# The first expert's weights: halves behind four tiles in place of whole units behind two

## The chip, the cores and the metric

The kernel runs on one core of a Trainium2 chip. The metric is the device time of one execution in microseconds (us), the median of several executions. TensorE (PE) multiplies matrices, VectorE (DVE) and ScalarE (ACT) work on elements, GpSimd (POOL) gathers rows, and SyncE (SP) issues nearly all DMAs. An engine runs its own instructions in the order in which they are written, and engines wait for each other and for DMAs on semaphores.

## The reference

Three blocks, one after the other; only the first and the beginning of the second bear on this change.

```python
    batch, n_heads, seq, head_dim = (4, 8, 576, 64)
    ...
    N, D, E, F = (2304, 512, 8, 1024)
    ...
    n_tokens, d_model, d_ff = (2304, 512, 1536)
    ...
    scores = scale * np.matmul(q, k.transpose(0, 1, 3, 2))
    gamma = 1.0 - 2.0 ** (-5.0 - np.arange(H, dtype=np.float32))
    ...
    Dmat = np.where(rel >= 0, gamma[:, None, None] ** rel[None, :, :], 0.0)
    ret = scores * Dmat[None, :, :, :]
    return np.matmul(ret, v).astype(np.float32)
...
    logits = x @ w_gate
    e_idx = np.argmax(logits, axis=1)
    ...
    for e in range(E):
        ...
        h = np.maximum(x[mask] @ w1[e], 0.0)
        ye = h @ w2[e]
        out[mask] = gate_w[mask, None] * eom[mask, e, None] * ye
...
    a = x @ w_a
    b = x @ w_b
    return (a * b @ w_out).astype(np.float32)
```

All data are float32. `w1` of one expert is 512 x 1024 (2 MB), `w2` of one expert 1024 x 512 (2 MB).

## The kernel before

**Stage 1 (about 0 to 112 us): decay attention and routing.** The 576 positions of each of the B = 4 batches are cut into C = 5 tiles: four of 128 rows and a last one of 64. Tile c of batch b is written (b, c) here. For each tile, SP loads q, k and v (pieces of 256 bytes, two DMAs each for q and k and one for v), DVE scales q and k by powers of the decay (`scale_qk`), PE turns them (`turn_qk`), multiplies them (`score`), DVE masks (`probs`), PE multiplies by v (`mix`) and carries a state to the next tile. The result x of the tile is turned back by `turn_x` together with the gate logits (`keep_logits` on DVE), copied to `x_tok` by ACT (`keep_x`) and stored to `x_tokens` in HBM by SP (`store_tile`). Batch 0 is written out; SP runs the loads of batches 1 to 3 in a loop over b = 0, 1, 2 which in each turn, for each c, stores (b, c), waits until `mix` of (b, c) is done (the buffers of tile c come free then), and loads (b + 1, c). The last batch's stores stand behind the loop. At tile (b, c), DVE scales (b, c + 2) and PE turns (b, c + 1), so the loads of a tile have some three tiles of time from their release to their use.

**The first expert's weights.** The expert that runs first is always expert 0, so that its 4 MB can be loaded during stage 1 into `land[0]`: 8 units of 512 KB, of which units 0 to 3 (kind 0) are w1 and units 4 to 7 (kind 1) are w2. `load_first(kind, i)` (called from line 616 on, the DMA is put down to line 598) waits until the load before it of the same kind has landed, by the semaphores `first_in`, and issues unit i of that kind. In turn b, a unit of w1 goes behind the loads of tile (b + 1, 3) and one of w2 behind those of (b + 1, 4); the last unit of each kind goes behind the loop and ahead of the last batch's stores. ACT rounds each unit to `w_hi` and DVE subtracts it to `w_lo` (`first_low`). The table `first_units` says where: ACT copies unit 0 in (1, 1), unit 4 in (1, 3), 1 and 5 in batch 2, and in the last batch unit 2 in (3, 1), 3 in (3, 2), 6 in (3, 3) and 7 at the very end of the stage. In a tile, this copy is ACT's last work, and the next instruction behind it is the copy of the next tile's turned q (`qT`, line 912), for which PE waits in `turn_x`.

**Stage 2 (121 to 347 us)** runs windows of tokens through the experts, with the next expert's weights loaded meanwhile; **stage 3 (to the end)** is the two-factor block with seven products for eight. Neither is touched. PE is busy in both almost all the time.

Of the kernel before, what the change touches and what calls it, by code (L numbers as in the profile page):

```python
# [35 lines left out]
def retention_moe_bilinear(nc, q, k, v, w_gate, w_output_gate, w1, w2, w_a, w_b, w_out, out):  # L36
# [11 lines left out]
    P = 128  # L48
    B, H, S, DH = q.shape
    D = H * DH  # L50
    N = B * S
    E, _, F = w1.shape
    F2 = w_a.shape[1]
    DC = D // P
# [4 lines left out]
    C = -(-S // P)  # L59
# [48 lines left out]
    UNIT = 1024  # L108
# [17 lines left out]
    with ctx:  # L126
# [6 lines left out]
        def sem(name):  # L133
            return ctx.enter_context(nc.semaphore(name))
# [38 lines left out]
        land = []  # L173
# [239 lines left out]
        first_in = [sem("first_up_in"), sem("first_down_in")]  # L413
# [69 lines left out]
        def after(b, c, n):  # L483

            return b + (c + n) // C, (c + n) % C

        def first_units(b, c, first, last):


            if first:  # L490
                return None
            if last:
                return {1: (2, 4), 2: (3, 5), 3: (6, 6)}.get(c)
            return {1: (b - 1, b * 2 - 2), 3: (b + (DC - 1), b * 2 - 1)}.get(c)
# [71 lines left out]
        def _(sp):  # L566
            from_q_k_v = ((q, q_in, q_in_done), (k, k_in, k_in_done), (v, v_in, v_in_done))

            def load_tile(b, c, which=from_q_k_v):
                r = ROWS[c]  # L570
                for src, dst, done in which:
                    rows = src.rearrange("b h s d -> s b h d")[c * P:c * P + r, bass.ds(b, 1)]
                    to = dst[0:r, c, :].rearrange("s (b h d) -> s b h d", b=1, h=H)
                    if src is v:
                        sp.dma_start(to, rows).then_inc(done[c], 16)  # L575
                    else:

                        for half in range(2):
                            sp.dma_start(to[:, :, half:H:2, :], rows[:, :, half * HP:half * HP + HP, :]).then_inc(done[c], 16)  # L579

            def store_tile(b, c):
                r = ROWS[c]
                sp.wait_ge(x_ready, b * C + (c + 1))
                sp.dma_start(x_dram[bass.ds(b * S + c * P, r), :], x_tok[0:r, c, :]).then_inc(x_stored[c], 16)

            def load_first(kind, i):

                sp.wait_ge(first_in[kind], i * 16 + 16)  # L590
                sp.sem_inc(alone_sp, 1)
                if kind == 0:
                    src = w1.rearrange("e (d p) f -> p (e d) f", p=P)[:, bass.ds(i, 1), :]
                    dst = land[0][:, bass.ds(i, 1), :]
                else:
                    src = w2.rearrange("e (g two p) n -> p (e g) two n", p=P, two=2)[:, bass.ds(i, 1), :, :]
                    dst = land[0][:, bass.ds(i + DC, 1), :].rearrange("p u (g n) -> p u g n", g=2)
                sp.dma_start(dst, src).then_inc(first_in[kind], 16)


# [8 lines left out]
            with sp.Fori(0, B - 1) as b:  # L609
                for c in range(C):  # L610

                    store_tile(b, c)
                    sp.wait_ge(mixed, b * C + (c + 1))
                    load_tile(b + 1, c)
                    if c >= C - 2:
                        load_first(c - (C - 2), b)
            for kind in range(2):
                load_first(kind, B - 1)
            for c in range(C):
                store_tile(B - 1, c)  # L620

# [286 lines left out]
        def _(act):  # L908
            def turn_qk(b, c):
                r = ROWS[c]  # L910
                act.wait_ge(q_turned, b * C + (c + 1))
                nc.scalar.copy(qT[:, c, :, 0:r], pq[:, :, 0:r]).then_inc(qT_ready, 1)
                act.wait_ge(k_turned, b * C + (c + 1))
                nc.scalar.copy(kT[:, c, :, 0:r], pk[:, :, 0:r]).then_inc(kT_ready, 1)

            def keep_state(b, c):
                act.wait_ge(state_done, b * (C - 1) + (c + 1))
                nc.scalar.copy(state[:], pstate[:]).then_inc(state_kept, 1)

            def keep_xT(b, c):  # L920
                r = ROWS[c]
                act.wait_ge(mixed, b * C + (c + 1))
                nc.scalar.copy(xT[:, :, 0:r].rearrange("p (h n) t -> p h n t", h=2), pout[:, :, 0:2, 0:r]).then_inc(xT_ready, 1)


            def keep_x(b, c):
                r = ROWS[c]
                act.wait_ge(logits_kept, b * C + (c + 1))
                act.wait_ge(x_stored[c], b * 16 + 16)
                for h, bank in enumerate(x_banks(b, c)):  # L930
                    ins = nc.scalar.copy(x_tok[0:r, c, 2 * h * P:2 * (h + 1) * P].rearrange("p (i n) -> p i n", i=2),
                                         bank[0:r, 0:2 * TURNED].rearrange("p (i n) -> p i n", i=2)[:, :, 0:P])
                ins.then_inc(x_ready, 1)
# [12 lines left out]
            def batch(b, first, last):  # L946
                for c in range(C):
                    if not (last and c == C - 1):
                        turn_qk(*after(b, c, 1))
                    if not (first and c == 0) and not (last and c == C - 1):  # L950
                        keep_x(*after(b, c, -1))
                    if c < C - 1:
                        keep_state(b, c)
                    keep_xT(b, c)
                    if last and c == C - 1:
                        keep_x(b, c - 1)
                    unit = first_units(b, c, first, last)
                    if unit:
                        u = unit[0]
                        if last:  # L960
                            act.wait_ge(first_in[u // DC], 16 * (u % DC) + 32)
                        else:
                            act.wait_ge(first_in[c // 3], b * 16 + 16)
                        act.sem_inc(alone_act, 1)
                        nc.scalar.copy(w_hi[0][:, bass.ds(u, 1), :], land[0][:, bass.ds(u, 1), :]).then_inc(hi_done, 1)

            batches(act, batch)
            keep_x(B - 1, C - 1)
            act.wait_ge(first_in[1], 16 * DC + 16)
            nc.scalar.copy(w_hi[0][:, UE - 1, :], land[0][:, UE - 1, :]).then_inc(hi_done, 1)  # L970


# [1177 lines left out]
```

## Time and profile before

| | |
|---|---|
| median of 3 runs | 775.74 us (773.78 to 776.17) |
| profiled execution | 770.1 us |
| its span, first to last instruction | 768.1 us |
| mean granted clock of TensorE | 0.995 of full speed |
| busy share of the span: PE, DVE, ACT, POOL | 98%, 63%, 36%, 10% |
| DMA, mean over the span | 220 GB/s, 168.81 MB |
| DMA, 0 to 160 us | 35.97 MB in 68445 packets, 59284 of them under 512 bytes |

The profile is one execution; its own time of 770.1 us is the span and 2.0 us around it. A row of the timeline below gives start, duration, engine, line, operation and tiles, the count of merged instructions, and in brackets how long the engine stood idle before it and whom the profile puts that down to. An instruction of SP that issues a DMA is shown with the time that the issue takes, not the transfer.

### The profile page before, as it was taken

How to read it: one execution, taken by the hardware profiler on the slowest of the kernel's cores; microseconds unless marked ns; L12 is line 12 of the kernel's file. 1: busy time of each engine (PE TensorE's matmuls, PEld its weight loads, DVE VectorE, ACT ScalarE, POOL GpSimd, SP SyncE). 2: the span in 40 equal slices, each digit the busy share in tenths (PEclk: the TensorE clock that was granted, in tenths of full speed). 3: DMA queues.
4: the chain of work that ended last, by engine and by line, in shares of the span. 5: the costliest groups of instructions: out<-in, count | busy, mean ns of one | idle time of the engine just before them, and what ended most of it. 6: DMA issues, size and time to landing. Idle time of an engine off the chain costs nothing.

```text
span 768.1 us, 14705 instructions
## 1 busy us (share of the span) xinstructions
PE 754.7 (98%) x5370; PEld 702.2 (91%) x5370; DVE 481.0 (63%) x925; ACT 275.8 (36%) x500; POOL 78.7 (10%) x108
## 2 busy tenths in 40 slices
PE   9999999999999999999999999999999999999996
PEld 6888868999999999999899999999999999999994
DVE  5678886577576676666567787547654555544371
ACT  4454543465464554533132343211321221221021
POOL 2000032101101110100011100301110030111003
PEclk9999999999999999999999999999999999999998
DMA  9989927397788789587732767875444476444402
GB/s 172 229 231 247 240 98 226 124 357 261 258 321 297 237 296 337 189 327 278 307 128 80 261 257 292 300 285 204 158 189 153 190 260 233 168 175 173 170 1 82
DMA packets 116630, 168.81 MB, mean 220 GB/s; under 512 B 63981, under 2 KB 83472, under 8 KB 116560
## 3 DMA queue, kind: packets, MB, share of 16 engines
q1 hardware_dynamic: 111149, 156.90, 60.4%
q0 software_dynamic: 4176, 10.92, 4.5%
q8 instruction: 41, 0.67, 0.4%
q10 hardware_dynamic: 1234, 0.07, 0.1%
q14 instruction: 30, 0.24, 0.1%
HBM read 131.34 MB, written 36.54 MB: 219 GB/s over the span
## 4 chain that ended last, share of the span: by engine, by line
PE 88%; SPq 5%; issue 2%; DVE 2%; DMA 1%; ACT 1%; POOL 0%; POOLq 0%; DVEq 0%; ACTq 0%
PE pz L2079 34%; PE po L2104 19%; PE py L2024 14%; PE pu L2013 9%; SPq L579 4%; PE pu L1995 4%; PE pu L2003 2%; PE px L1966 1%; PE pscore L1780 1%; PE pout L1850 1%; SPq L575 1%; PE pq L1803 1%; PE pk L1803 1%; PE pstate_bank L1836 1%; DMA x_blk<-x_tokens,slots 1%
## 5 line engine op out<-in xcount | busy, mean ns | idle before, releaser
L2079 PE MATMUL pz<-x_hi,w_hi 128*128 128x384 f32 x504 | 170.4, 338 | 0.3 <-DVE u L1639 0.3
L2079 PE MATMUL pz<-x_hi,w_lo 128*128 128x384 f32 x504 | 170.0, 337 | 0.0
L2079 PE MATMUL pz<-x_lo,w_hi 128*128 128x384 f32 x504 | 169.7, 337 | 0.0
L1639 DVE TENSOR_TENSOR u<-pz,p 128x384 f32<-128x384 f32 x72 | 40.1, 558 | 115.4 <-PE pz L2079 115.4
L2079 PEld LDWEIGHTS pz<-x_hi,w_hi 128*128 128x128 f32 x504 | 94.6, 188 | 3.3 <-DVE u L1639 0.6
L2079 PEld LDWEIGHTS pz<-x_lo,w_hi 128*128 128x128 f32 x504 | 94.8, 188 | 0.7
L2079 PEld LDWEIGHTS pz<-x_hi,w_lo 128*128 128x128 f32 x504 | 94.8, 188 | 0.0
L1080 ACT COPY p<-pz 128x384 f32<-128x384 f32 x36 | 17.3, 480 | 212.7 <-PE pz L2079 212.7
L2104 PE MATMUL po<-wo_hi,g_hi 128*128 128x512 f32 x216 | 84.3, 390 | 0.0
L2104 PE MATMUL po<-wo_hi,g_lo 128*128 128x512 f32 x216 | 84.3, 390 | 0.0
L2104 PE MATMUL po<-wo_lo,g_hi 128*128 128x512 f32 x216 | 84.2, 390 | 0.0
L2024 PE MATMUL py<-h_hi,w_hi 128*128 128x320 f32 (+6 forms) x256 | 80.2, 313 | 0.0
L2024 PE MATMUL py<-h_hi,w_lo 128*128 128x320 f32 (+6 forms) x256 | 77.5, 303 | 0.0
L2024 PE MATMUL py<-h_lo,w_hi 128*128 128x320 f32 (+6 forms) x256 | 77.4, 303 | 0.0
L1539 DVE TENSOR_TENSOR w_lo<-land,w_hi 128x1024 fp32r<-128x1024 f32 x56 | 68.5, 1223 | 10.7 <-ACT w_hi L1005 10.3
L1005 ACT CAST w_hi<-land 128x1024 fp32r<-128x1024 f32 x56 | 58.7, 1048 | 0.2 <-DMA land<-in_moe_w_dram 0.2
L2013 PE MATMUL pu<-x_hi,w_hi 128*128 128x320 f32 (+6 forms) x160 | 49.3, 308 | 0.0
L1095 ACT CAST g_hi<-g 128x384 fp32r<-128x384 f32 x72 | 33.6, 514 | 43.2 <-DVE g L1662 39.9
L2013 PE MATMUL pu<-x_lo,w_hi 128*128 128x320 f32 (+6 forms) x160 | 48.5, 303 | 0.0
L2024 PEld LDWEIGHTS py<-h_lo,w_hi 128*128 128x128 f32 x256 | 48.4, 189 | 0.0
L2013 PE MATMUL pu<-x_hi,w_lo 128*128 128x320 f32 (+6 forms) x160 | 48.4, 302 | 0.0
L2104 PEld LDWEIGHTS po<-wo_hi,g_lo 128*128 128x128 f32 x216 | 40.6, 188 | 8.5
(261 smaller groups left out, 1318.8 us busy)
## 6 DMA issues: line engine op xcount, KB each, us to landing
land<-in_moe_w_dram SPq DMA_DIRECT2D x64, 512.0 KB, 7.6
w_hi<-bilinear_weights SPq DMA_DIRECT2D x31, 896.0 KB, 4.6
w_lo<-bilinear_weights SPq DMA_DIRECT2D x31, 896.0 KB, 7.0
bilinear_weights<-w_hi SPq DMA_DIRECT2D x12, 896.0 KB, 10.1
bilinear_weights<-w_lo SPq DMA_DIRECT2D x12, 896.0 KB, 11.4
wo_land<-in_moe_w_out_dram SPq DMA_DIRECT2D x18, 512.0 KB, 3.9
q_in<-in_q_dram SPq DMA_DIRECT2D x32, 128.0 KB, 3.2
k_in<-in_k_dram SPq DMA_DIRECT2D x32, 128.0 KB, 3.3
```

What stands on the lines that cost most here:

```text
L579: sp.dma_start(to[:, :, half:H:2, :], rows[:, :, half * HP:half * HP + HP, :]).then_inc(done[c], 16)
L1005: nc.scalar.copy(w_hi[1 - s][:, u, :], land[1 - s][:, u, :]).then_inc(hi_done, 1)
L1080: nc.scalar.copy(p1[:], pz[n % 2][:, 0:T]).then_inc(z_kept_act, 1)
L1095: nc.scalar.copy(hi[:, MADE[i], :], g[:, MADE[i], :]).then_inc(g_hi_ready, 1)
L1539: nc.vector.tensor_tensor(w_lo[1 - s][:, u, :], land[1 - s][:, u, :], w_hi[1 - s][:, u, :], ALU.subtract).then_inc(lo_done, 1)
L1639: nc.vector.tensor_tensor(dst, pz[n % 2][:, 0:T], more, ALU.add).then_inc(z_kept_dve, 1)
L1803: last = nc.tensor.matmul(banks[h][0:r, second * P:second * P + TURNED], xT[:, d, 0:r], turn_w[:, h, (1 - second) * LG:(1 - second) * LG + ...
L1995: last = nc.tensor.matmul(pu[f][:, cols_of], w[s][:, d, at(f)], x_hi[:, d, cols_of], start=(d == 0 and w is w_hi), stop=False)
L2013: last = nc.tensor.matmul(pu[f % NPU][:, cols_of], w, m[:, d, cols_of], start=(d == 0 and n == 0), stop=(d == DC - 1 and n == 2))
L2024: last = nc.tensor.matmul(py[d][:, cols_of], w, m[:, f, cols_of], start=(f == 0 and n == 0), stop=(f == FF - 1 and n == 2))
L2079: ins = nc.tensor.matmul(pz[n % 2][:, 0:T], w, m, start=(k in FRESH and j == 0 and i == 0), stop=(j == DH2 - 1 and i == 2), skip_group_che ...
L2104: ins = nc.tensor.matmul(po[i][:], m[:, c, rows], w_, start=(q == 0 and f == 0 and n == 0), stop=(q == NQ - 1 and f == 1 and n == 2))
```

## The change

`load_first` gets a third argument and fetches half a unit: of a w1 unit the left or right 512 of its 1024 columns (so 2 KB a row in place of 4 KB), of a w2 unit one of its two groups of 128 rows (2 KB a row, as before). The halves of the two kinds of turn b go behind the loads of the tiles (b + 1, 1), (b + 1, 2), (b + 1, 3) and (b + 1, 4), and the last units follow behind the loop as four halves. Each half still waits for the one before it of its kind, so the second half of a unit now waits for the first half to land. The counts for which ACT waits are adapted; when and in which order ACT and DVE work on the units stays the same.

```diff
--- before.py
+++ after.py
@@ -585,16 +585,17 @@
 
 
 
-            def load_first(kind, i):
-
-                sp.wait_ge(first_in[kind], i * 16 + 16)
+            def load_first(kind, i, half):
+
+                sp.wait_ge(first_in[kind], i * 32 + (16 * half + 16))
                 sp.sem_inc(alone_sp, 1)
                 if kind == 0:
-                    src = w1.rearrange("e (d p) f -> p (e d) f", p=P)[:, bass.ds(i, 1), :]
-                    dst = land[0][:, bass.ds(i, 1), :]
+                    cols = slice(half * (UNIT // 2), (half + 1) * (UNIT // 2))
+                    src = w1.rearrange("e (d p) f -> p (e d) f", p=P)[:, bass.ds(i, 1), cols]
+                    dst = land[0][:, bass.ds(i, 1), cols]
                 else:
-                    src = w2.rearrange("e (g two p) n -> p (e g) two n", p=P, two=2)[:, bass.ds(i, 1), :, :]
-                    dst = land[0][:, bass.ds(i + DC, 1), :].rearrange("p u (g n) -> p u g n", g=2)
+                    src = w2.rearrange("e (g two p) n -> p (e g) two n", p=P, two=2)[:, bass.ds(i, 1), half, :]
+                    dst = land[0][:, bass.ds(i + DC, 1), :].rearrange("p u (g n) -> p u g n", g=2)[:, :, half, :]
                 sp.dma_start(dst, src).then_inc(first_in[kind], 16)
 
 
@@ -612,10 +613,11 @@
                     store_tile(b, c)
                     sp.wait_ge(mixed, b * C + (c + 1))
                     load_tile(b + 1, c)
-                    if c >= C - 2:
-                        load_first(c - (C - 2), b)
+                    if c >= 1:
+                        load_first((c - 1) // 2, b, (c - 1) % 2)
             for kind in range(2):
-                load_first(kind, B - 1)
+                for half in range(2):
+                    load_first(kind, B - 1, half)
             for c in range(C):
                 store_tile(B - 1, c)
 
@@ -958,15 +960,15 @@
                     if unit:
                         u = unit[0]
                         if last:
-                            act.wait_ge(first_in[u // DC], 16 * (u % DC) + 32)
+                            act.wait_ge(first_in[u // DC], 32 * (u % DC) + 48)
                         else:
-                            act.wait_ge(first_in[c // 3], b * 16 + 16)
+                            act.wait_ge(first_in[c // 3], b * 32 + 16)
                         act.sem_inc(alone_act, 1)
                         nc.scalar.copy(w_hi[0][:, bass.ds(u, 1), :], land[0][:, bass.ds(u, 1), :]).then_inc(hi_done, 1)
 
             batches(act, batch)
             keep_x(B - 1, C - 1)
-            act.wait_ge(first_in[1], 16 * DC + 16)
+            act.wait_ge(first_in[1], 32 * DC + 16)
             nc.scalar.copy(w_hi[0][:, UE - 1, :], land[0][:, UE - 1, :]).then_inc(hi_done, 1)
 
 
```

On SP, at the loads of tile (b + 1, 2) in the loop, the order before is this: line 575 is the v load that ends a tile (here of tile 1), line 584 the store of the next tile's x, and lines 579 and 575 its loads.

```order
L575 DMA v_in<-in_v_dram 128x8x64
L583 REGISTER_ALU
L584 ISA [waits x_ready]
L584 DMA x_tokens<-x_tok 128x512
L579 ISA [waits mixed]
L579 DMA q_in<-in_q_dram 128x4x64
L579 ISA
L579 DMA q_in<-in_q_dram 128x4x64
```

The order after, at the same place:

```order
L575 DMA v_in<-in_v_dram 128x8x64
L590 ISA
L599 ISA [waits first_up_in]
L599 DMA land<-in_moe_w_dram 128x512
L583 REGISTER_ALU
L584 ISA [waits x_ready]
L584 DMA x_tokens<-x_tok 128x512
L579 ISA [waits mixed]
L579 DMA q_in<-in_q_dram 128x4x64
L579 ISA
```

Behind tile 1's v load now stand a wait for `first_up_in` and a DMA of 128 x 512 into `land`, ahead of the store and the loads of tile 2. The same is inserted behind tile 2; the halves behind tiles 3 and 4 take the places of whole units there.

At the end of the loop and behind it, the order on SP before was this (line 598 is the weights' DMA, line 584 with x4 and x1 the last batch's five stores):

```order
L575 DMA v_in<-in_v_dram 64x8x64
L598 ISA [waits first_down_in]
L598 DMA land<-in_moe_w_dram 128x2x512
L609 REGISTER_ALU
L609 COMPARE_AND_BRANCH
L598 DMA land<-in_moe_w_dram 128x1024 [waits first_up_in]
L598 DMA land<-in_moe_w_dram 128x2x512 [waits first_down_in]
L584 DMA x_tokens<-x_tok 128x512 [waits x_ready] x4
```

The order after, at the same place:

```order
L575 DMA v_in<-in_v_dram 64x8x64
L599 ISA [waits first_down_in]
L599 DMA land<-in_moe_w_dram 128x512
L610 REGISTER_ALU
L610 COMPARE_AND_BRANCH
L599 DMA land<-in_moe_w_dram 128x512 [waits first_up_in] x2
L599 DMA land<-in_moe_w_dram 128x512 [waits first_down_in] x2
L584 DMA x_tokens<-x_tok 128x512 [waits x_ready] x4
```

Behind the loop there are now four DMAs with a wait each in place of two; the second and the fourth wait for the one just ahead of them, and the last batch's stores stand behind all four.

## Rows read from the trace of the kernel before

**Rows 1.** The page's first part: busy time, share, instructions of TensorE.

```profile
PE 754.7 (98%) x5370; PEld 702.2 (91%) x5370; DVE 481.0 (63%) x925; ACT 275.8 (36%) x500; POOL 78.7 (10%) x108
```

**Rows 2.** Timeline of SP's queue, 32 to 97 us.

```profile
32.70 0.38 SPq L575 DMA_DIRECT2D v_in<-in_v_dram  x1
33.35 0.37 SPq L584 DMA_DIRECT2D x_tokens<-x_tok  x1
33.90 1.04 SPq L579 DMA_DIRECT2D q_in<-in_q_dram  x2
...
36.13 0.46 SPq L575 DMA_DIRECT2D v_in<-in_v_dram  x1
36.97 1.61 SPq L598 DMA_DIRECT2D land<-in_moe_w_dram  x1
38.84 0.59 SPq L584 DMA_DIRECT2D x_tokens<-x_tok  x1
...
46.38 1.56 SPq L579 DMA_DIRECT2D k_in<-in_k_dram  x2
...
60.99 0.46 SPq L575 DMA_DIRECT2D v_in<-in_v_dram  x1
61.82 0.68 SPq L598 DMA_DIRECT2D land<-in_moe_w_dram  x1
62.77 0.58 SPq L584 DMA_DIRECT2D x_tokens<-x_tok  x1
...
70.18 1.17 SPq L579 DMA_DIRECT2D k_in<-in_k_dram  x2
...
91.93 4.66 SPq L598 DMA_DIRECT2D land<-in_moe_w_dram  x3
```

**Rows 3.** Table by stretches, 42 to 44 us: busy time of each engine, PEclk, DMA share, GB/s.

```profile
42.00:44.00 2.00, 2.00 (x36) 1.71 (x33) 1.82 (x9) 2.00 (x5) 0.00 (x0) 1.00 0.46 106
```

**Rows 4.** Timeline of DVE, scaling of k for (1, 3) and (3, 0).

```profile
39.89 0.69 DVE L1169 TENSOR_TENSOR k_in<-k_in,powers 128x512 f32<-128x512 f32 x1 [0.22 <-DMA k_in<-in_k_dram]
...
75.72 0.69 DVE L1169 TENSOR_TENSOR k_in<-k_in,powers 128x512 f32<-128x512 f32 x1
```

**Rows 5.** Chain of waits: start, duration, what (loads of k for (2, 0)).

```profile
46.98 4.04 DMA k_in<-in_k_dram
```

**Rows 6.** Timeline of PE: turns of (1, 3), (2, 0), and `turn_x` of two tiles.

```profile
42.57 0.66 PE L1768 MATMUL pq<-ident,q_in 128*128 128x128 f32 x4
...
53.17 0.65 PE L1768 MATMUL pq<-ident,q_in 128*128 128x128 f32 x4 [0.79 <-ACT x_tok L931]
...
55.23 0.73 PE L1803 MATMUL pq<-turn_w,xT 128*128 128x144 f32 x4 [0.58 <-ACT qT L912]
...
99.58 0.76 PE L1803 MATMUL pq<-turn_w,xT 128*128 128x144 f32 x4
```

**Rows 7.** Timeline of ACT in (1, 1), and at the end of (3, 2).

```profile
41.16 0.37 ACT L931 COPY x_tok<-pq 128x256 f32<-128x256 f32 x1 [2.60 <-DVE logits L1212]
...
98.00 1.05 ACT L965 CAST w_hi<-land 128x1024 fp32r<-128x1024 f32 x1
98.96 0.37 ACT L912 COPY qT<-pq 128x256 f32<-128x256 f32 x1
```

**Rows 8.** DMA issues: us to landing; first issue behind (3, 4), 91.9 us.

```profile
land<-in_moe_w_dram SPq DMA_DIRECT2D x1, 512.0 KB, 4.2
```

**Rows 9.** The same for the issue at 92.6 us, unit 3.

```profile
land<-in_moe_w_dram SPq DMA_DIRECT2D x1, 512.0 KB, 4.7
```

**Rows 10.** The same for the issue at 96.2 us, alone in the queue.

```profile
land<-in_moe_w_dram SPq DMA_DIRECT2D x1, 512.0 KB, 3.9
```

**Rows 11.** DMA issues, 33 to 36 us: the v load of (1, 2).

```profile
v_in<-in_v_dram SPq DMA_DIRECT2D x1, 256.0 KB, 3.0
```

**Rows 12.** Waits of SP's queue, 17 to 115 us, at a store and at a weight load.

```profile
SPq L584 <- ACT x_tok L931: 11.7, 7, 4.1
...
SPq L591 <- DMA land<-in_moe_w_dram: 3.1, 1, 3.1
```

## Prediction

> **What bounds the kernel now.** I read the page first: PE is busy 98% of the span [rows 1], so only a place where PE stands still, or will stand still, can change the time. The edit touches stage 1 alone, so I then read the chain of waits up to 121 us. The reader should see two regimes there. Up to about 51 us the chain runs through SP's queue and ends in the landing of a k load of tile (2, 0), issued at 46.98 and landed 4.04 us later [rows 5]. From there on the chain is PE itself. PE's timeline shows what the first regime costs: the turn of (2, 0) starts after 0.79 us of idling and the next `turn_x` after 0.58 us [rows 6], 1.37 us together. These are the largest gaps of PE in the four batches. Third, SP's timeline: the queue hardly ever stands still, and the loads of a tile come late after their release. Fourth, the table by stretches: the DMA engines stand half empty behind the short fifth tile of turn b = 0 (share 0.46 at 42 to 44 us) [rows 3]. The whole w1 unit goes out just ahead of that short tile, so before the change its bytes flow where SP feeds the DMA engines least.
>
> **The price of one more weight DMA on SP.** From a v load to the next store SP needs 0.27 us where no weights stand between (32.70 + 0.38 to 33.35). With a unit between them it is 1.32 us in turn b = 1 (60.99 + 0.46 to 62.77) and 2.25 us in turn b = 0 (36.13 + 0.46 to 38.84) [rows 2]. So a weight DMA takes 1.05 to 2.0 us of the queue. For a half I take 1.0 us: a half has the same number of rows, and the issue depends little on the bytes (0.68 us for a w1 unit, 0.46 us for a v load with half the bytes [rows 2]). By bytes a half costs nearly the same: 0.26 MB at the 220 GB/s of the profile's mean is 1.2 us of full DMA engines. Either way the loads of tile 2 come 1.0 us later in each turn and those of tile 3 2.0 us later. For (b + 2, 0), a turn's four halves stand ahead in place of two units: 2.0 us later if SP's issue is the limit, not later if the bytes are (they are the same). I take the middle, 1.0 us.
>
> **What that does to PE, turn b = 0.** Tile (1, 3): its k was waited for by DVE even before (0.22 us of idling, start 39.89 [rows 4]), so it has no slack and DVE is 2.0 us later. Behind `scale_qk` on DVE stands `keep_logits` of (1, 0), and behind that ACT's `x_tok`, 41.16 us, two copies, done at 41.16 + 0.27 + 0.38 = 41.81 (the second copy is taken to start 0.27 us behind the first and to last 0.38, an estimate from its form); PE's turn of (1, 3) at 42.57 [rows 6, 7] waits for it. Of 2.0 us, 0.76 us are slack, so PE loses 1.24 us. Then (2, 0): 1.0 us later, which is less than PE is late already, so the old gap of 1.37 us is kept and not widened. Front: **+1.2 us**. Its bounds: below, -1.4 us, if the shorter backlog ahead of (2, 0) (a half in place of a unit) brings its k early and tile 3 costs nothing; above, +3.1 us: SP loses the full 2.0 us in each of the first two turns, 4.0 us at (3, 0), whose second k load was issued by 70.18 + 1.17/2 = 70.77, landed at about 74.8 with the 4.04 us of rows 5, and was used at 75.72 [rows 2, 4], 0.9 us of slack. In turn b = 2 and behind the loop SP has caught up and waits for x itself (7 waits, 11.7 us in all [rows 12]), so there a lateness of SP dies away.
>
> **The last w1 unit, behind the loop.** Here the halves are strictly in series. Before, three units were issued from 91.93 on; the first landed after 4.2 us, the second (unit 3, issued at 92.6) after 4.7 us, at 97.3 [rows 2, 8, 9], 0.7 us before ACT starts to copy it at 98.00 [rows 7]. SP already waited once, 3.1 us, for the unit ahead [rows 12]; the stores behind it came out in time, and the new waits delay those of (3, 0) and (3, 1) only, while POOL's gather waits for the last one, so I price these at nothing (if the cover were gone, up to one landing, 3 us). Afterwards: unit 3's first half is issued at about 92.6, with just a half ahead of it. It lands after 3.0 us at best (the v load of the same 256 KB [rows 11]) and 4.2 us at worst [rows 8]; I take 3.5. Only then is the second half issued, and it lands after 3.0 us (3.9, the row of a whole unit alone in the queue, is the upper bound [rows 10]). 92.6 + 3.5 + 0.1 + 3.0 = 99.2, so ACT waits 1.2 us (bounds 0.7 and 2.8). Queued behind this copy on ACT is the turned q of (3, 4), which ended at 98.96 + 0.37 = 99.33 [rows 7]; PE's `turn_x` of (3, 2), 99.58 [rows 6], waits for it, 0.25 us of slack. PE loses **0.95 us** (bounds 0.4 and 2.5), and from here to the gather the chain has no slack that could give it back. Unit 7 is needed 10 us later than unit 3 and is hidden.
>
> The Trainium skill (DMA: Bandwidth & Descriptors, "Anatomy of one DMA") puts a fixed 2.0 us on each DMA of the gpsimd path and adds the bytes at 436 GB/s, and its rules for authors ask to coalesce small transfers. That speaks against the change, as two halves in series pay the fixed part twice. By its figures a half lands in an estimated 2.6 us, 99.2 would become 97.9, the term of 0.95 us would vanish and the sum would be +1.2 us. The rows here are slower for both sizes (3.0 and 3.9 us, on SP's queue), so I stay with them.
>
> **The sum.** Stages 2 and 3 get the same instructions and only start later. 1.24 + 0.95 = +2.2 us; 770.1 us of the profiled execution become 772.3 us. The median before is 775.74 us, 5.6 us above that execution; I put the difference on the median, and shade it to +2.0 us because PE may pick up a little of it in gaps such as those before the last gather: **777.7 us**.
>
> **The rivals.**
> *Both costs at their upper ends (slower).* SP's issue is the limit in all turns, so the front costs 3.1 us, and the tail 1.5 us, with landings near 4 and 3.3 us: +4.6 us, 780.3 us. For it: the chain runs through SP's queue; against it: the stretched issues (1.61 and 1.56 us [rows 2]) look like an SP held up by full DMA queues, which absorbs extra issue time. It decides where (2, 0) and (3, 0) are more than 1 us later than now.
> *Hidden (no change).* The slack around DVE and ACT absorbs the front, or the halves land in 2.7 us each and ACT does not wait: 0 to +1.2 us, 775.7 to 776.9 us. It is also the rule of the skill for the tail. For it: PE stands still for only 1.37 us where loads are late; against it: no landing under 3.0 us is in the rows for this size.
> *The gap at 53 us closes (faster).* Weights spread over four tiles leave (2, 0) less to queue behind, the two gaps go, and the rest is hidden: -1.4 us, 774.3 us. For it: k of (2, 0) took 4.04 us to land right behind a whole w2 unit. Against it: all bytes ahead of it are the same, and DMA engines half empty at 42 to 44 us [rows 3] show that the unit had little to push. Beyond -0.3% it comes only if loads wait longer in the plain executions (5.6 us slower than the profiled one) than in the trace.
>
> **How the numbers follow.** A measurement of this kernel can tell about 0.3%, 2.3 us. My forecast, costs near the middle (+0.5 to +3.5, 776.2 to 779.3 us, for it alone): 0.45, of which 0.25 falls within the bound and 0.20 above. The slower rival 0.22, all above. Hidden 0.17, all within. The gap closes 0.16, of which 0.09 below the bound and 0.07 within. Together: faster 0.09, same 0.49, slower 0.42. The range for 8 in 10 reaches down to the faster rival less some spread of a median, 773.8, and up to the slower one, 780.5.
>
> **What the changed profile would show.** SP: the store behind tiles 1 and 2 comes 1.0 us later behind v than before; the loads of (1, 3) start at about 36 instead of 33.90 us; the DVE idles about 2 us before the k of (1, 3), and PE's turn of that tile comes 1.2 us late. Two waits of about 3 us each stand behind the loop for the weights. ACT idles about 1.2 us before its copy of unit 3, put down to that DMA, and PE idles about 1 us before `turn_x` of (3, 2). The first window starts 2 us later, and all after it has equal length. The prediction is wrong if the loads of (1, 3) are not late (then SP was held up by the queues), if ACT does not wait for unit 3, or if stage 2 or 3 changes in length.

## The result and the profile after

The changed kernel takes 778.17 us (774.2 to 782.0, 12 runs) against 773.1 us of the kernel before in the same series; the ratio is 1.0077, 95% interval [1.0056, 1.0098]. By the ratio it is slower by 6.0 us, [4.3, 7.6]; the two medians lie 5.1 us apart. In a second series (below) it was 1.0062 [1.0036, 1.0089], 4.8 us.

First the page of the changed kernel, its span (768.1 us before):

```profile
span 776.6 us, 14736 instructions
```

The span is 8.5 us longer. Where these come in is found by following one and the same instruction through both traces. PE's timeline of the kernel before at four places: `turn_x` of (3, 1) and (3, 3), one small matmul near the end of stage 1 (line 1857, `hot_now`; line 1859 in the changed kernel), and the first matmul of stage 2.

```profile
94.74 0.76 PE L1803 MATMUL pq<-turn_w,xT 128*128 128x144 f32 x4
...
103.64 0.76 PE L1803 MATMUL pq<-turn_w,xT 128*128 128x144 f32 x4
...
109.19 0.17 PE L1857 MATMUL plog<-hot_now,before 128*128 128x8 bf16 x1 [0.93 <-DVE hot_now L1346]
...
121.13 0.41 PE L1995 MATMUL pu<-x_hi,w_hi 128*128 128x320 f32 x1
```

The same timeline of the changed kernel: the turn of (1, 2), `turn_x` of (3, 1), (3, 2), (3, 3), the `hot_now` matmul, and the first matmul of stage 2.

```profile
37.86 0.65 PE L1770 MATMUL pq<-ident,q_in 128*128 128x128 f32 x4 [1.21 <-ACT x_tok L933]
...
96.25 0.76 PE L1805 MATMUL pq<-turn_w,xT 128*128 128x144 f32 x4
...
104.03 1.30 PE L1805 MATMUL pq<-turn_w,xT 128*128 128x144 f32 x4 [2.88 <-ACT qT L914]
...
110.45 0.76 PE L1805 MATMUL pq<-turn_w,xT 128*128 128x144 f32 x4
...
116.00 0.17 PE L1859 MATMUL plog<-hot_now,before 128*128 128x8 bf16 x1 [0.93 <-DVE hot_now L1348]
...
127.89 0.41 PE L1997 MATMUL pu<-x_hi,w_hi 128*128 128x320 f32 x1
```

`turn_x` of (3, 1) comes at 96.25 in place of 94.74: the front has cost 1.5 us. `turn_x` of (3, 2) comes at 104.03 in place of 99.58 [rows 6]: 4.45 us late, 2.95 us more. `turn_x` of (3, 3) comes at 110.45 in place of 103.64: 6.81 us late, another 2.36 us. The first matmul of stage 2 starts 6.76 us late. The two causes behind the loop stand in the next views. The timeline of ACT, to be held against [rows 7]:

```profile
102.57 1.04 ACT L967 CAST w_hi<-land 128x1024 fp32r<-128x1024 f32 x1 [2.96 <-DMA land<-in_moe_w_dram]
103.52 0.37 ACT L914 COPY qT<-pq 128x256 f32<-128x256 f32 x1
```

ACT stands idle for 2.96 us before its copy of unit 3. The chain of waits says for what (start, duration, what):

```profile
95.66 4.07 DMA land<-in_moe_w_dram
...
99.80 2.67 DMA land<-in_moe_w_dram
```

The two landings of the halves stand in the chain one behind the other, 4.07 and 2.67 us. SP's queue waited twice behind the loop, 3.7 us for the first half of unit 3 and 2.5 us for the first half of unit 7 (us in total, times, longest; before it was one wait of 3.1 us [rows 12]):

```profile
SPq L591 <- DMA land<-in_moe_w_dram: 6.2, 2, 3.7
```

The other 2.36 us are in the table by stretches (columns: stretch, its length, then busy time of PE, PEld, DVE, ACT, POOL, granted clock, DMA share, GB/s):

```profile
102.00:104.00 2.00, 0.00 (x0) 0.00 (x0) 0.23 (x1) 1.43 (x3) 0.00 (x0) 0.84 0.31 119
104.00:106.00 2.00, 1.97 (x8) 1.94 (x8) 1.17 (x2) 0.16 (x1) 0.00 (x0) 0.50 0.76 222
...
110.00:112.00 2.00, 2.00 (x39) 1.88 (x39) 1.19 (x6) 0.63 (x1) 0.00 (x0) 0.95 0.00 0
```

Late in the gap of 2.88 us, at 103.4 us, the granted clock falls to 0.50, the lower of TensorE's two levels (1.2 GHz in place of 2.4 GHz), and it stays there until 110.2 us, 6.8 us in all. The `turn_x` row of 104.03 took 1.30 us where the one of 110.45 took 0.76.

The lateness that feeds the wait is in SP's timeline. Of the kernel before, the stores of (2, 0) and (2, 4):

```profile
68.40 0.36 SPq L584 DMA_DIRECT2D x_tokens<-x_tok  x1
...
86.68 0.58 SPq L584 DMA_DIRECT2D x_tokens<-x_tok  x1
```

Of the changed kernel, the half behind tile 2, the first loads of (1, 3), then the stores of (1, 0), (2, 0) and (2, 4), and the last half of the loop with the first one behind it (merged, x2):

```profile
34.07 0.36 SPq L599 DMA_DIRECT2D land<-in_moe_w_dram  x1
...
35.25 1.11 SPq L579 DMA_DIRECT2D q_in<-in_q_dram  x2
...
45.79 0.36 SPq L584 DMA_DIRECT2D x_tokens<-x_tok  x1
...
71.42 0.35 SPq L584 DMA_DIRECT2D x_tokens<-x_tok  x1
...
90.42 0.59 SPq L584 DMA_DIRECT2D x_tokens<-x_tok  x1
...
95.01 1.02 SPq L599 DMA_DIRECT2D land<-in_moe_w_dram  x2
```

The loads of (1, 3) start at 35.25 in place of 33.90 [rows 2]. The store of (2, 0) is 3.0 us late, that of (2, 4) 3.7 us, and the last half of the loop is issued at 95.01 where the last unit was at 91.93 [rows 2], 3.1 us late. In between, at the store of (2, 1), the lateness had shrunk to 2.1 us (75.01 against 72.95). SP's waits for x in the changed kernel, 17 to 125 us:

```profile
SPq L584 <- ACT x_tok L933: 9.8, 3, 5.8
```

All three stand behind the loop. In the kernel before, three of the seven waits of [rows 12] stand in turn 2, 2.3 us together.

DVE, scaling k of (1, 3), against [rows 4]:

```profile
41.79 0.69 DVE L1171 TENSOR_TENSOR k_in<-k_in,powers 128x512 f32<-128x512 f32 x1 [1.49 <-DMA k_in<-in_k_dram]
```

Here DVE waits 1.49 in place of 0.22 us. Of the remaining 1.7 us of the span, 1.43 are one wait of PE for a load of stage 3:

```profile
355.98 0.44 PE L2081 MATMUL pz<-x_hi,w_hi 128*128 128x384 f32 x1 [1.43 <-DMA w_lo<-bilinear_weights]
```

That one has nothing to do with the change; it stands in a second profile of the kernel before as well (last experiment).

### The profile page after: what moved, and what is told of

Same layout as the page of the kernel before. It is cut to its first block, busy times and chain, and to the rows that moved or that the text cites. A ratio compares the mean times of both kernels' runs of the same rounds, so it can differ in the third digit from the quotient of the medians.

```text
span 776.6 us, 14736 instructions
## 1 busy us (share of the span) xinstructions
PE 755.9 (97%) x5368; PEld 703.5 (91%) x5370; DVE 481.1 (62%) x925; ACT 275.8 (36%) x500; POOL 78.5 (10%) x108
## 4 chain that ended last, share of the span: by engine, by line
PE 80%; SPq 11%; DMA 4%; issue 2%; DVE 1%; POOL 0%; ACT 0%; POOLq 0%; DVEq 0%; ACTq 0%
PE pz L2081 33%; PE po L2106 19%; PE py L2026 12%; PE pu L2015 8%; SPq L579 6%; PE pu L1997 4%; PE pu L2005 2%; SPq L575 2%; DMA bilinear_weights<-w_lo 2%; SPq L599 1%; PE px L1968 1%; SPq L584 1%; DMA w_lo<-bilinear_weights 1%; DMA land<-in_moe_w_dram 1%; DMA x_blk<-x_tokens,slots 1%
```

## The experiments

The theory: two latenesses meet at unit 3. SP comes 3.1 us late to the end of the loop while PE is 1.5 us late, and the two halves in series take longer to land than one unit. ACT's wait makes PE stand, and the clock falls. The rivals: one of the two alone is the cause; half transfers as such are slow; the clock's fall costs nothing. The first four ran on one chip (before 770.27 us, 27 runs), the next four on another (before 775.09 us, 34 runs).

**Whole units behind the loop, halves in it.** `load_last` issues one DMA for the whole last unit of a kind.

```diff
             for kind in range(2):
-                for half in range(2):
-                    load_first(kind, B - 1, half)
+                load_last(kind)
```

> Halves behind four tiles in the loop as in the changed kernel, but whole units behind the loop as before. Theory (the two serial halves of unit 3 make ACT wait 3.0 us, PE stands 2.9 us, and the granted clock falls to 0.50 behind it; together 5.3 of the 6.8 us by which the first window starts late): ACT does not wait for unit 3, turn_x of (3, 2) follows without a gap, clock 1.00 there, and only the loss of turns 0 and 1 stays, +1.5 us over before. Rival (the halves in the loop make SP late everywhere, and the tail only shows it): still +5 us or more.

Ratio 1.0022 [1.0008, 1.0036], +1.7 us. The time is near what the theory said, the profile is not: ACT still waits for unit 3, 1.39 us.

```profile
100.21 1.04 ACT L979 CAST w_hi<-land 128x1024 fp32r<-128x1024 f32 x1 [1.39 <-DMA land<-in_moe_w_dram]
```

In this trace SP's lateness is enough to make ACT wait: unit 3 was issued at 95.31 us, 2.7 us later than before, and landed after 4.80 us, as long as before (4.7 [rows 9]). PE stood 1.30 us and the clock stayed at 1.00 behind it.

**Halves in series behind the loop, whole units in it.** Here `load_last` issues a half, behind a wait for the half before.

```diff
             for kind in range(2):
-                load_first(kind, B - 1)
+                for half in range(2):
+                    load_last(kind, half)
```

> The loop as before (whole units behind tiles 3 and 4), only the last unit of each kind behind the loop in two halves, each waiting for the one before. Theory: ACT waits 2 to 3 us for unit 3, PE stands as long, the clock falls to 0.50 for some 7 us, +5 us over before. Rival (loop is the cause): within 1 us of before.

Ratio 1.0022 [1.0005, 1.004], +1.7 us; neither 5 nor, by its profile, nothing. ACT and PE in its timelines:

```profile
99.12 1.04 ACT L980 CAST w_hi<-land 128x1024 fp32r<-128x1024 f32 x1 [1.42 <-DMA land<-in_moe_w_dram]
```

```profile
100.58 0.73 PE L1818 MATMUL pq<-turn_w,xT 128*128 128x144 f32 x4 [1.33 <-ACT qT L927]
```

Here the halves of unit 3, issued from 92.17 us on, landed after 4.11 and 2.65 us; ACT waited 1.42 us, PE stood 1.33 us, and the clock stayed at 1.00. My theory that the tail is nearly all of it falls: each part alone costs 1.7 us, 3.4 us together, where the whole change costs 4.8 to 6.0 us. What is missing could be what only the long gap brings, the clock; the intervals are wide enough that the sum alone does not show it.

**The changed kernel, the last halves not in series.** With the fourth argument, `load_first` signals that semaphore and has no wait ahead.

```diff
+        last_in = [sem("last_up_in"), sem("last_down_in")]
...
-                    load_first(kind, B - 1, half)
+                    load_first(kind, B - 1, half, last_in[kind])
```

> As the changed kernel, but the halves behind the loop signal semaphores of their own, so that none waits for the one before; same bytes, same 2 KB rows, same four DMAs. Theory (the wait in series is the cost, not the size of a half): unit 3 lands within 1 us of before, no wait of ACT over 0.5 us, +1.5 us over before, like the run with whole units behind the loop. Rival (halves as such move slower, or four issues cost too much of SP): ACT still waits 2 us or more, +4 us or more.

Ratio 1.0034 [1.0018, 1.0049], +2.6 us. SP issues the five DMAs behind the last loads in 2.37 us (8.55 in the changed kernel), and still ACT waits 2.15 us:

```profile
95.57 2.37 SPq L601 DMA_DIRECT2D land<-in_moe_w_dram  x5
```

```profile
101.82 1.04 ACT L972 CAST w_hi<-land 128x1024 fp32r<-128x1024 f32 x1 [2.15 <-DMA land<-in_moe_w_dram]
```

Half of the rival is right: with five DMAs issued together unit 3 has not landed much sooner, at 101.7 in place of 102.5 us. But by the ratios 2 to 3 us of the loss are gone. In the traces the gap is 0.8 us shorter (2.07 in place of 2.88 us), and the clock stayed at 1.00.

**The changed kernel with PE kept busy**, twice, the second time beside the changed kernel on one chip.

```diff
+                    if last and c == C - 2:
+                        keep_busy(10, plog[:])
                     if not (first and c == 0):
                         turn_x(*after(b, c, -1))
```

> As the changed kernel, with ten matmuls of zeros (128 x 512, bf16, about 0.29 us each) ahead of turn_x of (3, 2), which fill the time in which PE waits for ACT. Theory (of the loss behind the loop, 2.3 us are the clock that falls when PE stands still): ACT still waits 3 us, but the clock stays at 1.00 from 100 to 112 us, the first window starts about 2.3 us earlier than in the changed kernel, +4.5 us over before. Rival (the clock's fall costs nothing that shows, or falls anyway): as the changed kernel, +6 to +7 us.

> The changed kernel with ten matmuls of zeros ahead of turn_x of (3, 2), again, now on one chip with the changed kernel. If the fall of the clock takes its time in the plain executions too: 2 to 3 us faster than the changed kernel of this call. If it does not occur in most of them, or costs nothing: the same as the changed kernel within 1 us.

> The changed kernel as it is, on the same chip as the three runs below, as their second yardstick beside the kernel before. Theory by now: SP reaches the end of the loop 3 us late (about 95 in place of 91.9 us), the two halves of unit 3 in series add 1.4 us, ACT waits 3 us, the clock falls to 0.50 behind it; +6 to +7 us over before. If the fall of the clock is a matter of a narrow margin, the profile may also show it at 1.00 with a wait of 2 to 3 us, and the time then is +4 to +5 us.

In the first call: 1.0068 [1.0055, 1.0081], +5.2 us [4.2, 6.2], from five runs, with the clock at 1.00 from 100 to 112 us in its profile. That is between the theory's 4.5 and the rival's 6 us, on a chip on which the changed kernel itself was not run; it decides nothing. In the second call: changed kernel 780.15 us, 1.0062 [1.0036, 1.0089]; kept busy 777.25 us, 1.0041 [1.0018, 1.0064]; by the ratios 1.6 us apart, by the medians 2.9. ACT waited for unit 3 in all of them: 2.96 and 3.89 us in the two profiles of the changed kernel, 3.41 and 2.97 us in the two kept busy. The changed kernel's PE in the second call and its table by stretches:

```profile
105.38 0.73 PE L1805 MATMUL pq<-turn_w,xT 128*128 128x144 f32 x4 [3.81 <-ACT qT L914]
...
116.57 0.17 PE L1859 MATMUL plog<-hot_now,before 128*128 128x8 bf16 x1 [0.94 <-DVE hot_now L1348]
```

```profile
106.00:108.00 2.00, 2.00 (x23) 1.72 (x24) 1.23 (x7) 0.65 (x2) 0.00 (x0) 0.51 0.95 324
```

With PE kept busy:

```profile
103.70 0.73 PE L1805 MATMUL pq<-turn_w,xT 128*128 128x144 f32 x4 [0.62 <-ACT qT L914]
...
113.29 0.17 PE L1859 MATMUL plog<-hot_now,before 128*128 128x8 bf16 x1 [0.93 <-DVE hot_now L1348]
```

```profile
106.00:108.00 2.00, 1.68 (x42) 1.33 (x39) 1.02 (x4) 1.61 (x3) 0.00 (x0) 1.00 0.65 243
```

In both profiles of the changed kernel the clock fell, with gaps of 2.88 and 3.81 us; in both with the matmuls of zeros, where gaps of 1.06 and 0.62 us were left, it did not. What the fall costs is read between two fixed instructions, from `turn_x` of (3, 2) to the `hot_now` matmul: 11.97 us (104.03 to 116.00) and 11.19 us (105.38 to 116.57) with the fall, 9.59 us (103.70 to 113.29) without, and 9.58 to 9.61 us in every other profile on record. So in the traces the fall costs 2.4 and 1.6 us; it lasted 6.8 us in the first and 3.4 us in the second. Up to the first matmul of stage 2 the difference is larger, 23.86 and 22.95 us against 20.68 and 20.85 us (124.65 - 103.97 and 124.55 - 103.70), but the rest of it goes with the wait for the first gather, 1.30 and 1.34 us against 0.22 and 0.59 us, and this wait is 1.22 and 1.30 us too in the runs with the clock at 1.00 throughout (halves only behind the loop, halves not in series).

The plain runs of the second call do not show the cost of the fall: their intervals overlap, and the difference may be nothing or as large as in the traces. The mean granted clock of these runs, 0.9930 for the changed kernel, 0.9945 kept busy and 0.9942 before, points the same way, but it varies too much from run to run to settle it.

**The places of before, each unit as two DMAs.**

```diff
-                sp.wait_ge(first_in[kind], i * 16 + 16)
+                sp.wait_ge(first_in[kind], i * 32 + 16)
+                for half in range(2):
...
+                    sp.dma_start(dst, src).then_inc(first_in[kind], 16)
```

> The places of before (behind tiles 3 and 4, and behind the loop), but every unit as two DMAs of 256 KB issued one behind the other without a wait between. Same bytes at the same places, two DMAs more a turn on SP. If SP's issue is the limit (my first reason for the front): SP is 1 us later for each turn, about 2 to 3 us late at the end of the loop, PE loses 1 to 2 us at (2, 0), ACT waits 1 us or more for unit 3; +2 to +3 us. If the bytes and their place are the limit: within 1 us of before, and SP at the end of the loop at 91.9 to 92.9 us.

Ratio 1.0006 [0.9978, 1.0033]. SP's timeline, the stores of (1, 0) and (2, 0), and the end of the loop:

```profile
44.68 0.36 SPq L584 DMA_DIRECT2D x_tokens<-x_tok  x1
...
69.82 0.35 SPq L584 DMA_DIRECT2D x_tokens<-x_tok  x1
...
92.87 2.05 SPq L600 DMA_DIRECT2D land<-in_moe_w_dram  x4
```

Against 44.59, 68.40 and 91.93 us before: 0.1, 1.4 and 0.9 us late. The second profile of the kernel before (last experiment) has the end of the loop at 92.68 us itself, so the 0.9 us are hardly more than its own spread. Two more issues a turn are mostly absorbed, above all in turn 0, and `turn_x` at the old gap comes at 55.17 (55.23 before). The number of issues is the smaller part. Yet ACT waited for unit 3 here as well, and PE stood 1.35 us behind it, with no loss of time to be seen in the plain runs:

```profile
99.61 1.04 ACT L967 CAST w_hi<-land 128x1024 fp32r<-128x1024 f32 x1 [1.44 <-DMA land<-in_moe_w_dram]
```

**Whole units, the w1 unit behind tile 2 in place of tile 3.**

```diff
-                    if c >= C - 2:
-                        load_first(c - (C - 2), b)
+                    if c in (2, C - 1):
+                        load_first(c // (C - 1), b)
```

> Whole units as before, four DMAs fewer than the changed kernel, but the w1 unit behind tile 2 in place of tile 3. If the place is what costs the front (weights ahead of a full tile 3 in place of the short tile 4): the k of (1, 3) is late by 1 to 2 us, PE loses about 1.2 us there, SP is 1 us or more late at the end of turns 0 and 1; +1 to +2 us. If only the number of issues counts: within 0.5 us of before.

Ratio 1.0019 [0.9995, 1.0043], +1.5 us. The same places in SP's timeline, and PE at (1, 3):

```profile
45.08 0.38 SPq L584 DMA_DIRECT2D x_tokens<-x_tok  x1
...
70.44 0.38 SPq L584 DMA_DIRECT2D x_tokens<-x_tok  x1
...
94.20 1.06 SPq L598 DMA_DIRECT2D land<-in_moe_w_dram  x2
```

```profile
43.86 0.65 PE L1768 MATMUL pq<-ident,q_in 128*128 128x128 f32 x4 [0.91 <-ACT x_tok L931]
```

SP is 0.5, 2.0 and 2.3 us late with no DMA more than before, and PE has the gap at (1, 3), 0.91 us (in the changed kernel the gaps are 1.21 us at 37.86, 0.29 at 43.99 and 0.37 at 46.04). By these profiles the place ahead of a full tile is the larger part of SP's lateness; with the two more issues it comes to about the 3.1 us of the changed kernel. `turn_x` of (3, 1) is 1.3 us late too, so ACT waited only 0.44 us for unit 3 and PE 0.47 us. The interval of the ratio reaches just below 1: the loss of time itself is not shown.

**Both units of a turn behind tile 3.** (This and the next ran on a third chip, before 772.35 us, 23 runs.)

```diff
-                    if c >= C - 2:
-                        load_first(c - (C - 2), b)
+                    if c == C - 2:
+                        load_first(0, b)
+                        load_first(1, b)
```

> The kernel before with whole units, both of a turn behind tile 3's loads (ahead of the short tile 4), in place of one behind tile 3 and one behind tile 4. Theory (it is the place of the weights among the tiles that moves PE): the loads of (2, 0) no longer stand behind a w2 unit, the gap of 1.4 us of PE at 53 us goes, SP reaches the end of the loop with nothing left to issue ahead of unit 3, which lands 1 us earlier; -1 us against before. Rival (tile (1, 4) is late by the 2 us of the second unit, more than its slack): PE loses 0.5 to 1.5 us there; the same or +1 us.

Ratio 1.0015 [1.0, 1.0031], +1.2 us: the rival's size. PE's gaps in the front:

```profile
37.47 0.65 PE L1769 MATMUL pq<-ident,q_in 128*128 128x128 f32 x4 [0.96 <-ACT x_tok L932]
...
45.59 0.73 PE L1804 MATMUL pq<-turn_w,xT 128*128 128x144 f32 x4 [0.65 <-ACT qT L913]
```

The gap of 0.79 us at 53 us went, and 0.36 us are left of the 0.58 us behind it, but PE lost 0.96 and 0.65 us earlier. The 0.96 us cannot be put down to the edit: they stand before the turn of (1, 2), whose loads are issued before anything here differs from the kernel before, and the second profile of the kernel before has 0.47 us at this place. ACT did not wait for unit 3.

**The weights on GpSimd's queue**, gated by mix steps chosen to give about the old times; `load_first` stands in GpSimd's program and is issued by it:

```diff
-                    if c >= C - 2:
-                        load_first(c - (C - 2), b)
...
+            with pool.Fori(1, B - 1) as b:
+                for kind in range(2):
+                    pool.wait_ge(mixed, b * C + (C + 1 + kind))
+                    load_first(kind, b)
```

> The kernel before with the first expert's whole units issued from GpSimd's queue, which has no work in this stage, gated by the same mix steps; SP issues only tiles and stores. Theory (a weight DMA takes 1 to 2 us of SP's queue, and SP's lateness is what hurts): SP is 2 us ahead at (2, 0), the gap at 53 us goes, unit 3 lands well before 98 us; -1 us against before. Rival (the bytes are the limit, or these transfers land so much slower from this queue that ACT waits for a unit): within 0.5 us of before, or slower.

Ratio 1.0017 [0.9996, 1.0037]. PE's timeline, at the place of the old gap and at `turn_x` of (3, 2):

```profile
54.18 0.73 PE L1809 MATMUL pq<-turn_w,xT 128*128 128x144 f32 x4 [0.24 <-ACT qT L920]
...
99.56 0.73 PE L1809 MATMUL pq<-turn_w,xT 128*128 128x144 f32 x4 [0.93 <-ACT qT L920]
```

In this execution `turn_x` at the old gap comes 1.05 us earlier than before (55.23), with SP relieved of the weights and its store of (2, 0) 2.3 us earlier. Unit 3 came late instead, landing at 98.0 us, and the gain went at 99.56.

**The same with units 2 and 3 issued first** (a fourth chip, before 774.09 us, 23 runs):

```diff
+            pool.wait_ge(mixed, (B - 1) * C)
+            load_first(0, B - 2)
+            load_first(0, B - 1)
+            load_first(1, B - 2)
+            load_first(1, B - 1)
```

> As the run with the weights on GpSimd's queue, with units 2 and 3 issued first (gated by the last mix of batch 2) and units 6 and 7 behind them, so that unit 3 lands before ACT copies it. Theory: ACT does not wait for unit 3, no gap of PE over 0.3 us between 53 and 100 us, the first window starts at 120 us or a little earlier, 1 us before the kernel before; -1 us. Rival (what GpSimd's queue saves is given back at the first gather, whose DMA PE then waits for, or by slower landings): within 0.3 us of before.

Ratio 1.0033 [1.0009, 1.0057], slower than before. PE at the old gap, and at the first gather:

```profile
55.60 0.73 PE L1809 MATMUL pq<-turn_w,xT 128*128 128x144 f32 x4 [0.58 <-ACT qT L920]
...
122.18 0.60 PE L1979 MATMUL py<-ident,x_blk 112*128 112x112 f32 x4 [1.31 <-DMA x_blk<-x_tokens,slots]
```

ACT did not wait for unit 3, but the front had its gaps again (0.59 us at 37.27, 0.69 at 53.55, 0.58 at 55.60) although turns 0 and 1 are issued as in the run ahead, and the gather's wait was 1.31 us where the kernel before had 0.66. At the old gap the two profiles lie 1.4 us apart, on two chips. Why the whole is slower than before is not settled.

**The kernel before, a second profile.**

> The kernel before as it is, with a profile of its own. It tells whether the wait of PE at the start of stage 3 (1.4 to 3.1 us for the load of w_lo, in the profile of the changed kernel and of most variants, not in the first one of before) comes with the change. If it has nothing to do with it: it may appear here too; the first window starts at 121 us, ACT waits for unit 3 less than 0.3 us, and the time is that of before. If the change causes it: absent here.

Ratio 0.999 [0.9964, 1.0015]. The wait at the start of stage 3 is there (1.8 us), so the change does not cause it. But I had also written that ACT waits less than 0.3 us, and that was wrong. ACT at unit 3; then PE at `turn_x` of (3, 2) and at the start of stage 3:

```profile
100.88 1.04 ACT L965 CAST w_hi<-land 128x1024 fp32r<-128x1024 f32 x1 [2.67 <-DMA land<-in_moe_w_dram]
```

```profile
102.34 0.73 PE L1803 MATMUL pq<-turn_w,xT 128*128 128x144 f32 x4 [2.59 <-ACT qT L912]
...
352.52 0.44 PE L2079 MATMUL pz<-x_hi,w_hi 128*128 128x384 f32 x1 [1.84 <-DMA w_lo<-bilinear_weights]
```

In this execution of the kernel before, the whole unit took long to land, and ACT waited 2.67 us. The DMA issue of unit 3, us to landing, against 4.7 in [rows 9]:

```profile
land<-in_moe_w_dram SPq DMA_DIRECT2D x1, 512.0 KB, 7.4
```

So the kernel before has this wait in some executions, and the first profile, with unit 3 landed 0.7 us early, was a good one. A single profile with a wait of 1.4 us for unit 3, as in the two runs with one half of the change and in the pairs, therefore shows nothing by itself at this place; the ratios of the plain runs are the measure, and they are clear of 1 for the two halves and not for the pairs. What does stand out in the profiles is the whole change: its four waits of ACT, 2.96 to 3.89 us, are longer than all ten others (0 to 2.67 us), and the 2.67 us belong to one of the two slowest of twelve executions (776.84 us, median 772.38).

## Why the prediction was right, and where it fell short

The measured loss, 4.8 to 6.0 us, is well over the forecast of 2.0 us, though the time, 778.17 us, lies in the range and 0.5 us from the forecast of 777.7. That nearness is luck: the forecast stood on the median of three runs before, 775.74 us, and twelve runs gave 773.1 us. The direction, the places and the order of the mechanism were right; the size was not. "Slower" had 0.42, less than "same", and slower is what came.

- **The front, +1.24 us forecast:** 1.51 us measured at `turn_x` of (3, 1). It came by loads behind full tiles, as said, but most of it one tile earlier (1.21 us at (1, 2)). By ACT's copy of unit 2, the six profiles with halves in the loop are 0.7 to 2.0 us behind the first one of the kernel before (92.62 us); its second is 0.1 us behind. "The old gap of 1.37 us is kept and not widened" held in the sense that PE, already late, stands there only 0.45 us.
- **"I take 1.0 us" for an extra DMA on SP, and the middle for (b + 2, 0):** the lateness at the store of (1, 0) was 1.2 us, as taken. The split was off: in the profile of the pairs the issues alone cost 0.1 us in turn 0 and 1.3 in turn 1; in that of the units behind tile 2 the place costs 0.5 and 1.5.
- **The step that failed: "In turn b = 2 and behind the loop SP has caught up ..., so there a lateness of SP dies away".** It does not. SP was 3.0 us late at (2, 0), 2.1 at (2, 1), 3.7 at (2, 4) and 3.1 at the end of the loop. The reading of [rows 12] behind it was wrong: of the 11.7 us in which SP waits for x only 2.3 stand in turn 2, the rest behind the loop. The changed kernel used these 2.3 us up, for it has no such wait in the loop. A tile of turn 2 with a half behind it took SP 5.1 us (75.01 to 80.09 us), a little more than PE's tile (4.84 us from `turn_x` of (3, 1) to (3, 2) before), so nothing more is caught up. I had priced the tail with unit 3's issue "at about 92.6"; it was 95.66. The lateness of SP beyond PE's own, 3.1 - 1.5 = 1.6 us, adds to the forecast wait: 1.2 + 1.6 = 2.8 us, measured 2.96.
- **The series of halves, 3.5 + 0.1 + 3.0 us:** 4.07 and 2.67 us with 0.07 between, 6.8 in place of 6.6 us. The second is near the 2.6 us estimated from the Trainium skill (DMA: Bandwidth & Descriptors, "Anatomy of one DMA"), whose figures are for the gpsimd path; the first, with another half just ahead, is not. The rival in which both land in 2.7 us did not come about. The term alone, tested by halves only behind the loop: gap 1.33 us (0.95 forecast), time +1.7 us [0.4, 3.1].
- **The term that was missing: the clock.** That a long gap lowers the granted clock was in no sum. In the traces it costs 2.4 us in the first profile of the changed kernel and 1.6 us in the second; in the plain runs its cost is not shown.
- **"Stages 2 and 3 ... only start later"** held but for a wait that comes and goes in both kernels.

The sum as it was in the first trace: 1.51 front, 2.95 wait, 2.36 clock, together 6.8 us at `turn_x` of (3, 3), and 6.76 us at the first matmul of stage 2. The plain runs lost less, 4.8 to 6.0 us. The profiled execution of the changed kernel was an average one (778.39 us), but that of the kernel before, 770.1 us, was 3 us below its median of 773.1, so the difference of these two traces overstates the loss. How the loss of an average execution divides is open.

## What to carry to other kernels

When a queue that issues transfers is nearly as busy as the engines it feeds, a lateness put in early is given back only as far as the queue had waits of its own. Count these waits in the very stretch where you want them to absorb it (here 2.3 us, not 11.7), and price the transfer with the least slack with the late queue and not with its old times. Of a change with two small costs, ask whether they end in the same wait: here each alone cost 1.7 us, and together they cost 4.8 to 6.0 us and made PE stand for 2.9 and 3.8 us, where the clock fell. Splitting a transfer in two that wait for each other makes one landing into two. Take a second profile of the kernel before, ahead of reading a difference of 1 us out of one: here the same wait was 0 in one and 2.67 us in the other.

## What the runs showed of the hardware

The granted clock fell from 1.00 to 0.50 with gaps of PE of 2.88 and 3.81 us, and not with gaps of 1.30, 1.33, 1.35, 2.07 and 2.59 us at the same place. With the first it fell at 103.4 us, while PE still stood, and was low for 6.8 us; with the second it fell at 106.0 us, 0.6 us after PE had gone on, and was low for 3.4 us. In the kernel before the clock fell too, later, where most matmuls of PE are those on zeros that fill its time (`idle_in`): 0.50 from 112 to 114 us in its first profile, 0.58 and 0.57 from 114 to 118 us in its second; in the changed kernel it stood at 1.00 there. This later fall costs next to nothing: from the `hot_now` matmul to the first matmul of stage 2 it is 11.94 and 11.99 us with it, and 11.89 and 11.76 us without it in the changed kernel. Unit 3, 512 KB, that landed within 4.7 us in one execution of the kernel before took 7.4 us in another. Two DMAs of 256 KB issued together in place of one of 512 KB made no measurable difference to the time, 1.0006 [0.9978, 1.0033].
